# Windowed attention in front of two MLPs on one core: three-deep buffers, spans laid out on the host, score tiles on all four quadrants, and the inverse of the row sums on GpSimd

## The reference, cut to what matters

```python
k_sum = k.reshape(B, H, nb, 32, D).max(axis=3)      # 24 blocks
v_sum = v.reshape(B, H, nb, 32, D).mean(axis=3)
scores_l = scale * q @ k.T      # kept only where |i - j| < 16, else -1e9
scores_s = scale * q @ k_sum.T + log(32)
a = exp(concat(scores_l, scores_s) - max)
a = a / (sum(a) + 1e-09)
x = a @ concat(v, v_sum)        # then heads side by side: 1536 x 512
h = relu(x @ w_in); y = h * h @ w_out
h = y @ w2_in;      g = P(h) / (Q(h) + 1e-6); out = g @ w2_out
```

## Time and profile before

| what | value |
|---|---|
| median of three runs | 624.05 us (623.88 to 625.15) |
| profiled execution: its own time | 623.78 us |
| profiled execution: span, first to last instruction | 622.1 us |
| mean granted TensorE clock | 0.997 of full |
| busy: TensorE, VectorE, ScalarE, GpSimd | 594.0, 443.7, 262.2, 144.5 us |
| DMA loads for attention, each unit | k, q and vnat 384 KB each; vwin 384 KB and 2 x 88 KB; block means 144 KB |

### The profile page before, as it was taken

One profiled execution on the slowest core, in us unless ns is written; L12 is line 12 of the kernel. 1 busy time (PEld: TensorE's weight loads), 2 busy tenths in 40 slices (PEclk: granted clock), 3 DMA queues, 4 the chain that ended last, 5 costly groups with the idle time before them and its releaser, 6 DMA issues.

```text
span 622.1 us, 9784 instructions
## 1 busy us (share of the span) xinstructions
PE 594.0 (95%) x3264; PEld 486.2 (78%) x3264; DVE 443.7 (71%) x862; ACT 262.2 (42%) x553; POOL 144.5 (23%) x144
## 2 busy tenths in 40 slices
PE   5878989999999999999999989999999999999995
PEld 4766768888888888888888867778888888888884
DVE  5656679667343333356666599999999999999996
ACT  4757731111131111130111755556756666765663
POOL 5435450000030000030000465622222222222220
PEclk9989999999999999999999999999999999999999
DMA  8999856000000000022222300000100000100001
GB/s 239 232 196 239 182 194 249 0 1 0 1 0 0 0 0 0 0 68 99 82 92 100 101 1 0 1 0 1 68 0 0 0 0 0 68 0 1 0 1 67
DMA packets 26973, 35.54 MB, mean 57 GB/s; under 512 B 1856, under 2 KB 19264, under 8 KB 26944
## 3 DMA queue, kind: packets, MB, share of 16 engines
q1 hardware_dynamic: 24544, 33.96, 19.4%
q10 hardware_dynamic: 2400, 1.18, 0.9%
HBM read 30.80 MB, written 3.15 MB: 55 GB/s over the span
## 4 chain that ended last, share of the span: by engine, by line
PE 47%; DVE 35%; issue 11%; POOL 3%; DMA 1%; ACT 1%; DVEq 1%; POOLq 0%
PE bank L479 22%; PE bank L536 21%; DVE ratio L941 9%; DVE numer L923 6%; DVE ratio L935 5%; DVE numer L921 5%; DVE ratio L930 5%; DVE hhi L948 4%; POOL kwin L318 2%; PE bank L434 2%; POOL prob L340 1%; DMA vwin<-vsum 1%; PE bank L444 1%; PE bank L452 1%; PE bank L465 1%
## 5 line engine op out<-in xcount | busy, mean ns | idle before, releaser
L479 PE MATMUL bank<-xhi,whi 128*128 (+1 forms) x384 | 149.7, 390 | 1.2 <-DVE wlo L829 1.2
L479 PE MATMUL bank<-xlo,whi 128*128 (+1 forms) x384 | 149.4, 389 | 0.0
L479 PE MATMUL bank<-xhi,wlo 128*128 (+1 forms) x384 | 149.4, 389 | 0.0
L632 ACT ACTIVATE hsq<-bank 128x512 f32<-128x512 f32 x48 | 28.7, 598 | 218.6 <-PE bank L479 218.6
L394 POOL TENSOR_TENSOR denom<-denom,habs 128x512 f32<-128x512 f32 (+1 forms) x49 | 62.3, 1272 | 250.9 <-ACT denom L703 250.9
L479 PEld LDWEIGHTS bank<-xhi,whi 128*128 128x128 f32 x384 | 72.1, 188 | 16.3 <-DVE wlo L829 1.4
L479 PEld LDWEIGHTS bank<-xlo,whi 128*128 128x128 f32 x384 | 72.1, 188 | 15.0
L479 PEld LDWEIGHTS bank<-xhi,wlo 128*128 128x128 f32 x384 | 72.1, 188 | 15.0
L551 PE MATMUL bank<-whi,hhi 128*128 128x512 f32 x192 | 75.9, 395 | 7.6 <-DVE hlo L952 7.6
L536 PE MATMUL bank<-hhi,whi 128*128 128x512 f32 x192 | 74.8, 390 | 0.1
L551 PE MATMUL bank<-wlo,hhi 128*128 128x512 f32 x192 | 74.9, 390 | 0.0
(11 more groups left out here) (67 smaller groups left out, 889.2 us busy)
## 6 DMA issues: line engine op xcount, KB each, us to landing
wraw<-w SPq DMA_DIRECT2D x32, 512.0 KB, 3.6
kraw<-kT SPq DMA_DIRECT2D x8, 384.0 KB, 7.9
q<-qT SPq DMA_DIRECT2D x8, 384.0 KB, 5.4
vnat<-v SPq DMA_DIRECT2D x8, 384.0 KB, 7.0
vwin<-v SPq DMA_DIRECT2D x8, 384.0 KB, 5.7
out<-osb SPq DMA_DIRECT2D x12, 256.0 KB, 2.1
vwin<-v SPq DMA_DIRECT2D x16, 88.0 KB, 5.9
vwin<-vsum ACTq DMA_DIRECT2D x8, 144.0 KB
```

Of the source, the lines that this page charges most:

```text
L479: last = mm(hps[j % 2][:, :], W[a][:, j, kt * P:(kt + 1) * P], X[b][:, kt, bass.ds(CH * c, CH)], start=k == 0, stop=k == 3 * KT - 1)
```

## The change

- **Keys and values laid out on the host.** k comes with 16 zero columns on either side; v comes as `vw`, for each unit 96 x 12 x 128, every window's 96 rows ready, so one DMA per unit with 6 KB per partition fills rows 0 to 95 of `vwin`. `vnat` and its load are gone.
- **Three sets of buffers** (RING = 3) for q, kraw, kwin, vwin and ksum.
- **Block means from the windows**: 12 matmuls (x24) of a 96x32 weight, each of four blocks of 32 columns of the array in turn; the result lies in four blocks of partitions. ScalarE copies 128x128; four DMAs from SyncE's queue (no longer ScalarE's) spread it, behind the loads of that queue.
- **Scores**: windows of even and odd number go to different halves of the PSUM partitions, and heads to different banks, so the 8 matmuls address all four 64x64 parts of the array in turn.
- **PSUM**: scores take four banks, the transposes one instead of two (turn(G) then waits for the copy of group G-1), the outputs of two groups share one bank, and `x_hi`, `x_lo` run once per two groups on 128x512.
- **Guard and inverse** go from VectorE to GpSimd: an add on 128x4, and a tensor_tensor with the operation pow and a tile of -1, ahead of the multiplication.
- GpSimd builds the keys of unit n+2 in group slots 0 and 1 of unit n; the first unit's keys are built in three parts. GpSimd splits weight slot 2 in groups 20 and 21, ahead of normalise(22) and normalise(23).
- The first loops of VectorE, ScalarE, GpSimd and SyncE over units are unrolled. The first `square` of the MLP stands ahead of the last x_hi and x_lo.

```diff
+RING = 3
+def unit(j, h): return 2 * j + h
-    sps, tps, ops, vps = bank[4:6], bank[6:8], bank[0:2], bank[2]
+    sps, tps, ops, vps = [bank[2:4], bank[4:6]], bank[6], bank[0:2], bank[7]
...
 SyncE
+        def load_vwin(n):
+            if n >= RING:
+                sp.wait_ge(o_done, done(2, GPB * (n - RING + 1) - 1))
+            sp.dma_start(vwin[n % RING][0:KW, :, :], vw[n]).then_inc(vw_in[n % RING], 16)
+        def spread_summary(n):
+            sp.wait_ge(vsum_copied, n + 1)
+            for t in range(4):
+                rows = KW + 2 * GPB * t
+                sp.dma_start(vwin[n % RING][rows:rows + 2 * GPB, :, :],
+                             vsum[n % 2][32 * t:32 * t + 2 * GPB, :].unsqueeze(1).to_broadcast([2 * GPB, NW, P])
+                             ).then_inc(vsum_in[n % RING], 16)
+        load_k(0); load_q(0); load_k(1); load_vwin(0)
+        load_q(1); load_vwin(1); load_k(2); load_q(2)
...
+        spread_summary(0)
+        for n in range(NB):
+            if n + 2 < NB: load_vwin(n + 2)
+            if n + RING < NB:
+                load_k(n + RING)
+                load_q(n + RING)
+            if 2 <= n < 2 + EARLY: load_first(n - 2)
...
+            if n + 1 < NB: spread_summary(n + 1)
 GpSimd
         def normalise(G, r):
+            pool.wait_ge(exp_done, G + 1)
+            g.tensor_scalar(inverse[r][:, :], rowsum[r][:, :], 1e-9, None, ALU.add).then_inc(guard_done, 1)
+            pool.wait_ge(guard_done, G + 1)
+            g.tensor_tensor(inverse[r][:, :], inverse[r][:, :], minus[:, :], ALU.pow).then_inc(inv_done, 1)
             pool.wait_ge(inv_done, G + 1)
             g.tensor_tensor(prob[r][:, :, :], prob[r][:, :, :],
                             inverse[r][:, :].unsqueeze(2).to_broadcast([P, GU, COLS]), ALU.mult).then_inc(norm_done, 1)
...
+        for G in range(GROUPS):
+            n, gi = divmod(G, GPB)
+            if G + 1 < GROUPS: normalise(G + 1, (G + 1) % P_RING)
+            if n + 2 < NB:
+                if gi == 0: load_windows(n + 2)
+                elif gi == 1: spread_all(n + 2)
+            x = G - GROUPS + 4
...
+                if x < 2 * (EARLY - DVE_FIRST):
+                    split(half_slot(DVE_FIRST + x // 2, x % 2), w_hi_pool, x, w_early)
 TensorE
+        def scores(G):
...
+            for j in range(GU // 2):
+                for e in range(2):
+                    w = GU * gi + 2 * j + e
+                    for h in range(2):
+                        rows = slice(D * h, D * h + D)
+                        last = mm(sps[G % 2][h][QW * e:QW * e + QW, j * COLS:(j + 1) * COLS],
+                                  q[r][rows, QW * w:QW * w + QW], kwin[r][rows, w, :], start=True, stop=True)
+        def summary(n):
...
+            for j in range(GPB):
+                for t in range(4):
+                    last = mm(vps[32 * t:32 * t + 32, 0:P], means[:, j, :], vwin[n % RING][0:KW, GPB * t + j, :],
+                              start=j == 0, stop=j == GPB - 1)
+        def turn(G, r):
+            pe.wait_ge(norm_done, G + 1)
+            pe.wait_ge(probT_done, done(2, G - 1))
 VectorE
-        def guard(G, g):
-            dve.wait_ge(exp_done, G + 1)
-            d.tensor_scalar(guarded[g % P_RING][:, :], rowsum[g % P_RING][:, :], 1e-9, None,
-                            ALU.add).then_inc(guard_done, 1)
-        def invert(G, g):
-            dve.wait_ge(guard_done, G + 1)
-            d.reciprocal(inverse[g % P_RING][:, :], guarded[g % P_RING][:, :]).then_inc(inv_done, 1)
+        for G in range(GROUPS):
+            if G >= 2:
+                (x_lo if G % 2 else x_hi)(G // 2 - 1)
...
+            if G + P_RING < GROUPS: masked(G + P_RING)
```

More of the change, by code:

```diff
@@ L62, with unit, build @@
 P_RING = 3
+RING = 3
+NB = PAIRS * B
+XPAIRS = GROUPS // 2
+KP = S + 2 * BAND
+def unit(j, h):
+    return 2 * j + h
 def done(credits, i):
     return credits + i + 1
-def build(nc, qT, kT, v, w1, w2, coef_a, coef_b, out):
+def build(nc, qT, kT, vw, w1, w2, coef_a, coef_b, out):
     base = 16512
@@ L112, in build @@
     half = FT // 2 * SLOT * 4
[L113 to L121, removed]
+    places = [Area(W_HI + half), Area(W_LO + half)]
+    q, kraw, kwin, vwin = [], [], [], []
+    for r, (near, far) in enumerate([(0, 0), (1, 1), (1, 0)]):
+        q.append(places[near](f"q{r}", [P, S]))
+        kraw.append(places[near](f"kraw{r}", [P, KP]))
+        kwin.append(places[far](f"kwin{r}", [P, NW, COLS]))
+        vwin.append(places[far](f"vwin{r}", [COLS, NW, P]))
+    vsum = [places[0](f"vsum{i}", [P, P]) for i in range(2)]
+    ksum = [places[1](f"ksum{r}", [P, NBLK]) for r in range(RING)]
+    assert all(a.offset <= w + 2 * half for a, w in zip(places, (W_HI, W_LO)))
     area = Area(WORK)
@@ L132, in build @@
     rowsum = [area(f"rowsum{i}", [P, GU]) for i in range(P_RING)]
[L133 removed]
     inverse = [area(f"inverse{i}", [P, GU]) for i in range(P_RING)]
[L135 removed]
+    work_end = area.offset
     area = Area(WORK)
@@ L350, in split @@
             g.tensor_tensor(wlo[index], wraw[index], whi[index].bitcast(F32), ALU.subtract).then_inc(sem_lo, 1)
[L352 to L356, removed]
-        normalise(0, 0)
[L358 to L380, removed]
+        pool.wait_ge(k_in[0], 16)
+        for gi in range(GPB):
+            windows(0, GU * gi, GU * (gi + 1))
+            if gi == 0:
+                pool.wait_ge(ksum_done, GPB)
+            spread_max(0, GU * gi, GU * (gi + 1), 1)
+        load_windows(1)
+        normalise(0, 0)
+        spread_all(1)
+        for G in range(GROUPS):
+            n, gi = divmod(G, GPB)
+            if G + 1 < GROUPS:
+                normalise(G + 1, (G + 1) % P_RING)
+            if n + 2 < NB:
+                if gi == 0:
+                    load_windows(n + 2)
+                elif gi == 1:
+                    spread_all(n + 2)
+            x = G - GROUPS + 4
+            if x >= 0:
+                if x == 0:
+                    pool.wait_ge(w_first, 16 * EARLY)
+                if x < 2 * (EARLY - DVE_FIRST):
+                    split(half_slot(DVE_FIRST + x // 2, x % 2), w_hi_pool, x, w_early)
         def y_lo(c):
@@ L419, in _ @@
         pe.sem_inc(b_done, 2)
[L421 to L425, removed]
+        def scores(G):
+            n, gi = divmod(G, GPB)
+            r = n % RING
             if gi == 0:
-                pe.wait_ge(q_in[s], 16 * (it + 1))
-                pe.wait_ge(windows_ready, n + 1)
+                pe.wait_ge(q_in[r], 16 * (n // RING + 1))
+            pe.wait_ge(windows_ready, G + 1)
             pe.wait_ge(s_free, done(2, G - 2))
-            for u in range(GU):
[L431 to L435, removed]
-            last.then_inc(s_done, 1)
@@ L819, in x_lo @@
-        def x_lo(it, g):
-            dve.wait_ge(xhi_done, GPI * it + g + 1)
-            d.tensor_tensor(xlo[x_part(it, g)], ops[g % 2][:, 0:GU * QW].unsqueeze(1),
-                            xhi[x_part(it, g)].bitcast(F32), ALU.subtract).then_inc(xlo_done, 1)
+            for j in range(GU // 2):
+                pair = GU // 2 * (g % GPB) + j
+                edge = 0 if pair == 0 else 2 if pair == NW // 2 - 1 else 1
+                for h in range(2):
+                    u = unit(j, h)
+                    last = d.tensor_tensor_reduce(prob[g % P_RING][:, u, :], sps[g % 2][h][:, j * COLS:(j + 1) * COLS],
+                                                  mask[:, edge, :], -SCALE, LARGE, ALU.add, ALU.min,
+                                                  lowest[g % P_RING][:, u:u + 1])
@@ L834, in split_weights @@
             split(j, index - EARLY + DVE_FIRST)
-        def attention(it, final, first):
-            for g in range(GPI):
-                G = GPI * it + g
-                inverts = g + 1 < GPI or not final
-                scores = g + P_RING < GPI or not final
-                before = (it, g - 1) if g > 0 else (it - 1, GPI - 1)
-                splits = g > 0 or not first
-                if inverts:
-                    guard(G + 1, (g + 1) % GPI)
-                if splits:
-                    x_hi(*before)
-                if inverts:
-                    invert(G + 1, (g + 1) % GPI)
-                if not final:
-                    block_max(it + 1, g // GPB, g % GPB, 1)
-                if scores:
-                    masked(G + P_RING, (g + P_RING) % GPI)
-                if splits:
-                    x_lo(*before)
-                if final and GPB <= g < GPB + DVE_FIRST:
-                    dve.wait_ge(w_first, 16 * EARLY)
-                    split(g - GPB, g - GPB)
-        block_max(0, 0, 0, GPB, first=True)
-        make_mask()
-        masked(0, 0)
-        masked(1, 1)
-        guard(0, 0)
-        invert(0, 0)
-        block_max(0, 1, 0, GPB, first=True)
-        masked(2, 2)
-        attention(0, False, True)
-        with dve.Fori(1, PAIRS - 1) as it:
-            attention(it, False, False)
-        attention(PAIRS - 1, True, False)
-        x_hi(PAIRS - 1, GPI - 1)
-        x_lo(PAIRS - 1, GPI - 1)
```

(30 more changed lines are left out.)

344 lines of the change are left out of this document (150 added, 194 removed).

## The result

The changed kernel takes 631.98 us (median, 629.4 to 633.25) against 623.96 us before; ratio 1.0133, 95% interval 1.0094 to 1.0171. It is slower by 8.0 us, where 13 us less were forecast. The profiled execution took 632.28 us, with a span of 630.6.

What follows compares the result with a forecast made beforehand. Attention, bound by TensorE and its waits, would become GpSimd's at 7.25 us per three groups. 14.3 + 17 x 2.42 + 5 x 2.15 + 1.5 + 0.6, plus 1.5, put the first hidden tile at 69.8: 610.5 us, range 603 to 624.

Steps and rivals of the forecast that it cites:

- the term for the pow: GpSimd's normalise, every group: the four-column pow taken at 0.40 us, between bounds of 0.19 and 1.41 from other operations.
- The chance of 0.14 for the slower side: Rival on GpSimd: a pow above 1.1 us makes the kernel slower, 631 us at 1.41; chance 0.14.
- the formula: Attention with a pow of p us on GpSimd: first hidden tile at 59.2 + 22p, from p = 0.75 on.
- the turning point: GpSimd's pow time at which the first hidden tile would equal the old 83.08: p = 1.09 us.
- two terms of the sum: Attention's start and end: first output at 14.3 instead of 17.73, and 1.5 us for turn(22) behind GpSimd's weight split.
- the slack I had counted: End of attention: GpSimd's first weight split was given half a group of slack, leaving 1.5 us for turn(22).
- handovers: Attention: 1.5 us added for uneven handovers among three engines within 10% of each other.
- The rival of late spreads: Block-mean spreads late behind SyncE's loads stop TensorE, 3 to 5 us each; two or three give 618 to 622; chance 0.09.
- the column blocks do overlap: TensorE: four array parts in turn give scores 0.62 and summary 0.92 us; rival of no overlap 624 us, chance 0.04.
- The DMA's relief: Attention loads in 6 KB rows instead of 512 byte pieces: 5.8 us per unit at 360 GB/s, below GpSimd's 7.25.
- the formula of a unit: GpSimd's need per three groups: 6.05 + 3 p us for a pow of p us, 7.25 at the value taken.
- the three signs of being wrong: Pow above 1.1 us, TensorE waiting on GpSimd's product in every group, or a long lower clock after a pause.

Runs made afterwards that it cites:

- e: Changed kernel with the pow on 128x8 instead of 128x4, the further four columns holding 1: 642.09 us, ratio 1.0305 to the kernel before.
- b: Changed kernel with a multiplication in place of the pow on GpSimd, no inverse computed: 619.73 us, ratio 0.9938 to the kernel before.
- h: Changed kernel with guard and inverse on VectorE and the start reordered, first unit's values loaded before second unit's keys: 619.62 us, ratio 0.9949.
- a: Changed kernel with guard and inverse back on VectorE, all else kept: 619.28 us, ratio 0.9943; repeated 617.71 us, ratio 0.9919.
- g: Changed kernel with guard and inverse on VectorE and two of the four spread DMAs issued by ScalarE: 624.47 us, ratio 1.0037.
- k: Changed kernel with guard and inverse on VectorE and the spreads queued ahead of the k, q and weight loads: 626.72 us, ratio 1.0073.
- d: Changed kernel with GpSimd's two half-slot weight splits behind normalise(23): 628.17 us, ratio 1.0109 to the kernel before.

## Why the prediction was wrong, by its own steps

**The step that failed** is the term for the pow: 0.40 us taken, 1.04 measured. I placed it by its column count next to the fixed part of other two-input operations. By e, with its two assumptions, the pow is paid largely by the column, some 0.157 us for each, where an ordinary column costs 0.0022 (the slope of the two sizes in the earlier trace rows). The bounds, 0.19 and 1.41, held it. The chance of 0.14 for the slower side was too small for a number that no row supported. By the formula the pow moves the first hidden tile from 69.8 to 82.1, 12.3 us; and b, with 0.20 in its place, is 12.3 us faster than the changed kernel.

**The pow alone did not make the kernel slower.** At p = 1.04 the formula gave 82.1, that is still 1 us faster than before; the prediction put the turning point at 1.09. The other 8 us to 90.4 were two terms of the sum, and b, which is 3 to 4 us faster than before and not 9 to 13 (610 to 615 us expected), shows that something besides the pow was missing. The first output came at 18.68 instead of 14.3. Of these 4.4 us, 2.6 are the block means, copied at 13.1 instead of 10.5: the first summary began only at 11.28, behind the load of the values, as h shows, where that load comes one place earlier and the summary 2.5 us sooner. The other 1.8 lie between copy and output: SyncE issues the four spread DMAs from 13.14 to 16.4, 3.3 us, and I had costed their issue at nothing. And turn(22) waited 4.66 us, not 1.5. Some 1.9 of these 3.2 us are GpSimd's instructions beside VectorE's splits (its own split 3.15 us instead of 2.50, guard and pow 2.56 instead of 1.28); another 1.0 is the slack I had counted, which a group of 2.44 us on GpSimd no longer has. 68.3 + 1.5 (handovers) + 12.3 (pow) + 4.4 + 3.2 = 89.7, against 90.36.

**A term that was missing**: the first hidden tile took 4.52 us instead of 3.06, at the lower clock after that pause; from its start to the first sum are 12.0 us instead of 10.7. In the steady part, too, the lower clock made two of four units 0.4 and 0.9 us longer than the formula.

**The rival of late spreads** came true as well, behind the pow: kernel a runs at 8.1 us per unit on the average of its steady part (68.47 - 28.00 = 40.5 us for five units, one of them held up by late keys), where those without a late spread need 7.35 (25.66 to 33.02 in the repeat of a). I had 7.1 for TensorE and ScalarE. Those 5 us, and the first output at 19.24 instead of 14.3, are why a's first hidden tile comes at 78.3 and not at the 68 to 72 expected of it.

**Right**: scores in 0.57 us (0.62 forecast) and the summary's 24 instructions in 0.79 (0.92), so the column blocks do overlap; the summary of the kernel after, for one:

```profile
26.51 0.86 PE L464 MATMUL bank<-vwin,means 96*32 96x128 f32 x24
27.30 0.69 PE L490 MATMUL bank<-probT,vwin 120*64 120x64 f32 x16
```

The DMA's relief (0.95 to 0.59 busy) was right too, as were the MLPs' unchanged length, GpSimd as the place where it would fail, and the formula of a unit. Of the three signs of being wrong, the low clock came, TensorE's wait for GpSimd came in half of the groups (11 of 22), and the pow stayed just under its 1.1. By the Trainium skill, GPSIMD Engine Reference (Engine selection), two-input work is about twice as slow there as on VectorE. The traces agree for an ordinary operation on 128x512: 1.295 us on GpSimd, 0.698 on VectorE (its square in the profile after). But the measured pow is six times VectorE's reciprocal of the earlier trace rows, so that factor is not to be carried over to a pow.

## What to carry to other kernels

An operation that no row of the trace shows deserves an experiment or a wide chance, not a value near the cheap end; with 22 to 24 uses on an engine that is about to become the bound, half a microsecond decides the sign. The same step cost 3.8 us in an arrangement with slack and about 12 in one without: price it in the kernel that it will stand in. And when small DMAs replace one, count their issue (0.77 us each here) and what stands behind them on each queue: moving them cost more (g, k) than leaving them.

## What the hardware did that I had not expected

- pow on GpSimd: 1.037 us for 128x4, 1.666 for 128x8; a multiplication of 128x4 on the same tiles 0.202.
- Beside VectorE's split of a weight slot, GpSimd's pow took 1.99 (changed kernel) to 2.34 us (d) instead of 1.04, and its 128x480 multiplication 2.00 (d) instead of 0.99.
- Two DMAs on ScalarE's queue, right behind a wait for its own copy, kept the engine from its next copy for 1.7 us (g). In the kernel before, where the wait had long cleared, the issue of one (27.41, 0.82 us) ran beside the exponentials (from 27.81). Whether the wait or the number makes the difference was not tested.
